# Attention quarters of the next batch grouped 2 + 1 + 2 between the token-mixing groups, on one Trainium2 core

## The chip, the core and the metric

The kernel runs on one core of one Trainium2 chip. The metric is the device time of one execution in microseconds (us), as the median of several runs. The engines are TensorE (matmuls and transposes, its weight loads shown apart), VectorE, ScalarE, GpSimd, and SyncE, which issues the DMAs.

## The reference, cut to what matters

All arrays are float32: batch 8, 8 heads, 576 tokens, 64 channels a head, so 512 channels for a token.

```python
kv = einsum('bhsd,bhse->bhde', k, v)      # per head: k^T v, 64 x 64
out = einsum('bhsd,bhde->bhse', q, kv)
x = out / sqrt(mean(out**2, -1) + 1e-6) * g_norm        # -> (8, 576, 512)

theta = x @ w_theta
y = w_tok_r @ (x * cos(theta)) + w_tok_i @ (x * sin(theta))    # over the tokens
u = x + y
x2 = u + relu(u @ w_ch)

u2 = x2 + (relu(x2^T @ w_tok1) @ w_tok2)^T
return u2 + relu(u2 @ w_ch1) @ w_ch2
```

The change concerns the part down to x2.

## The kernel before, in words

The program has four phases. Phase a computes x2, one batch after the other; phases b, c and d compute the rest, and nothing in them is changed. The five engines run their own instruction lists in order and meet at semaphores. Each list is written out by hand in a function of phase a: `tensor`, `scalar`, `vector`, `gpsimd`, `sync`. What stands where in these lists is the schedule; there is no planner. Matmuls of two kinds occur: the large products run on operands that are split into a high and a low part (three products each, lines 43 to 45 and 367, 368, 373), and the attention and the transposes run on plain fp32 (a quarter's four matmuls have eight records in the profile, a transpose's four have four).

The 576 tokens of a batch are five tiles: four of 128 and one of 64. In what follows **quarter** j (0 to 4) is the attention of one such tile for all heads, `attend(n, j)`: four matmuls (line 312) into a PSUM bank `ps_out[j % 2]`, so quarters 0, 2 and 4 share one bank and 1 and 3 the other. It waits until `norm(n, j - 2)` has read its bank.

For batch b (1 to 6 are the steady ones, written once as a loop body on TensorE) TensorE does:
- `theta(b, 0..4)`: 4 x 12 matmuls and 8 for the last tile, and then `kv(b + 1)`.
- The first half of the token mixing, four groups of output at once, in five pairs of input tiles (`token_mix_first_half`). After the fourth pair comes quarter 0 of batch b + 1.
- Groups five to eight of the token mixing (`token_mix(b, g)`, g = 4 to 7), 27 products each, each followed by one quarter of batch b + 1: quarters 1, 2, 3, 4.
- Eight groups of channel mixing (`channel_mix(b, g)`), 12 products each; `x_transpose(b + 1, 0)` after g = 4 and `x_transpose(b + 1, 1)` after g = 6, the other three behind g = 7. Groups from g = 4 on wait until `relu_add(b, g - 4)` has emptied their bank (that is, `d_x2`).

A quarter is followed by this chain for each tile: `squares` on ScalarE (line 552) into the only `square` tile; `mean_square` on VectorE, a TENSOR_REDUCE (line 721) and a small TENSOR_SCALAR (line 725); the power -1/2 on GpSimd (`inverse_rms`, line 948); `norm` on VectorE (line 733), which reads the quarter's bank; the gain on GpSimd (line 956); later `x_transpose` on TensorE, `x_hi` on ScalarE (line 559) and `x_lo` on VectorE (line 744). `squares(n, j)` waits until the reduction of tile j - 1 has read the `square` tile.

Between these, VectorE does for each token-mixing group g of batch b a `residual(b, g)` (lines 790 and 792; it empties the group's bank and waits for the group to be done) and, once ScalarE has made the high part (`u_hi`, line 596), `u_lo(b, g)` (line 797); and for each channel-mixing group `relu_add(b, g)` (line 805). `turn_q` (line 715) transposes the queries of a later batch, `turn_x2` (line 815) the finished x2.

Of the kernel before, what the change touches and what calls it, by code (L numbers as in the profile page):

```python
# [65 lines left out]
def phase_a(ctx, nc, m, banks, q, k, v, g_norm, w_theta, w_tok_r, w_tok_i, w_ch, x2_dram, x2t_dram):  # L66
    B, H, S, D = q.shape
    DM = H * D
    NC = DM // P
    NJ = 4  # L70
# [3 lines left out]
    NG = 2 * NC  # L74
# [193 lines left out]
    def tensor(pe, nxt):  # L268
# [123 lines left out]
        def token_mix_first_half(b, first):  # L392


            pe.wait_ge(d_frac, NT * b + NJ)
            wait(pe, d_x2, NG * b)
            for pair in range(NT):
                token_mix_pair(b, pair, FIRST_HALF)
                if pair == (1 if first else NJ - 1):
                    attend(b + 1, 0)  # L400

        def token_mix(b, g):

# [81 lines left out]
        def body(b, first=False, more=True):  # L485
            if not first:
                for j in range(NT):
                    theta(b, j)
            if more:
                kv(b + 1)  # L490
                if first:
                    q_transpose(b + 1, 0)
            if first:
                pe.wait_ge(a_whi, 3)
                pe.wait_ge(a_wt, 2 * NT)
                pe.wait_ge(d_wt, 2 * NT + 1)
            if more:
                token_mix_first_half(b, first)
                if first:
                    q_transpose(b + 1, 1)  # L500
                for g in range(NC, NG):
                    token_mix(b, g)
                    attend(b + 1, g - 3)
                    if first and g < NG - 1:
                        q_transpose(b + 1, g - 2)
            else:
                token_mix_last()
            if first:
                pe.wait_ge(d_wlo, 3)
            for g in range(NG):  # L510
                channel_mix(b, g)
                if more and g == 4:
                    x_transpose(b + 1, 0)
                if more and g == 6:
                    x_transpose(b + 1, 1)
            if more:
                for j in range(2, NT):
                    x_transpose(b + 1, j)
# [14 lines left out]
    def scalar(act, nxt):  # L533
# [15 lines left out]
        def squares(n, j):  # L549
            act.wait_ge(p_out, NT * n + j + 1)  # L550
            wait(act, d_ss, NT * n + j)
            act.activation(square, ps_out[j % 2][:, :], ACT.Square).then_inc(a_sq, 1)  # L552
# [82 lines left out]
        def body(b, first=False, more=True):  # L635
            if first:

                for j in range(NT):
                    if j + 1 < NT:
                        x_hi(0, j + 1)  # L640
                    if j == NJ:
                        turn_left(0)
                    tok_weight_hi(NT + 1 + j)
                    if 1 <= j <= 3:
                        sines(0, j - 1)
                tok_weight_hi(2 * NT + 1)
                act.wait_ge(a_left, 4)
                act.activation(wtok[0][:, 2 * NJ, :], left_tok[:, :], ACT.Copy).then_inc(a_whi, 1)
                act.wait_ge(d_wlo, 2)
                z_hi(0, 0)  # L650
                sines(0, 3)
                z_hi(0, 1)
                q_copy(1, 0)
                z_hi(0, 2)
                z_hi(0, 3)
                act.wait_ge(s_raw[2], DMA)
                act.activation(wch[0][:, :, :], raw_ch[:, :, :], ACT.Copy).then_inc(a_whi, 1)
                sines(0, NJ)
                z_hi(0, NJ)
            else:  # L660
                sines(b, 0)
                z_hi(b, 0)
                sines(b, 1)
                sines(b, 2)
                z_hi(b, 1)
                sines(b, 3)
                turn_left(b)
                if more:
                    kv_copy(b + 1)
                z_hi(b, 2)  # L670
                z_hi(b, 3)
                sines(b, NJ)
                z_hi(b, NJ)
            if more:
                squares(b + 1, 0)
            for g in range(NG):
                u_hi(b, g)
                if first and g == 0:
                    q_copy(b + 1, 1)
                if more and g >= NC:  # L680
                    squares(b + 1, g - 3)
                    if first and g < NG - 1:
                        q_copy(b + 1, g - 2)
            if more:
                for j in range(NT):
                    x_hi(b + 1, j)
            else:
                nxt["weights_hi"](act)
                act.wait_ge(g_zlo, NK * B)
                act.wait_ge(d_z, 2 * NT * B)  # L690
                for piece in range(3):
                    nxt["x_hi"](act, 0, piece)
        body(0, first=True)
        for b in range(1, B - 1):
            body(b)
# [3 lines left out]
    def vector(dve, nxt):  # L699
# [155 lines left out]
        def body(b, first=False, more=True):  # L855
            if first:

                for j in range(NT):
                    if 2 <= j + 1 < NT:
                        x_lo(0, j + 1)  # L860
                    if j >= 2:
                        rotate(0, j - 2)
                    if j < 3:
                        fraction(0, j)
                        magnitude(0, j)
                    if j == NJ:
                        fraction(0, 3)
                        magnitude(0, 3)
                    tok_weight_lo(NT + 1 + j)
                tok_weight_lo(2 * NT + 1)  # L870
                dve.wait_ge(a_whi, 3)
                dve.tensor_tensor(wtok[1][:, 2 * NJ, :], left_tok[:, :], wtok[0][:, 2 * NJ, :].bitcast(F32),
                                  ALU.subtract).then_inc(d_wt, 1)
                kv_copy(1)
                rotate(0, 3)
                fraction(0, NJ)
                magnitude(0, NJ)
                rotate(0, NJ)
                dve.wait_ge(a_whi, 4)
                dve.tensor_tensor(wch[1][:, :, :], raw_ch[:, :, :], wch[0][:, :, :].bitcast(F32),  # L880
                                  ALU.subtract).then_inc(d_wlo, 1)
            else:
                for j in range(NJ):
                    fraction(b, j)
                    magnitude(b, j)
                    if j >= 1:
                        rotate(b, j - 1)
                rotate(b, NJ - 1)
                fraction(b, NJ)
                magnitude(b, NJ)  # L890
                if more:
                    for hp in range(EARLY_TURNS, HP):
                        turn_q(b + 1, hp)
                rotate(b, NJ)
            if first:
                dve.wait_ge(d_wlo, 3)
            if more:
                mean_square(b + 1, 0)
            for g in range(NG):
                if more and g > NC:  # L900
                    norm(b + 1, g - NC)
                residual(b, g)
                if g >= 1:
                    u_lo(b, g - 1)
                if more and g >= NC:
                    mean_square(b + 1, g - 3)
                if more and g == 2:
                    norm(b + 1, 0)
            u_lo(b, NG - 1)
            for g in range(NG):  # L910
                relu_add(b, g)
                if more and g > NC:
                    turn_x2(b, g - NC - 1, turned)
                if more and g == 0:
                    norm(b + 1, NT - 1)
                if 1 <= g <= EARLY_TURNS and 1 <= b < B - 2:
                    turn_q(b + 2, g - 1)
                if first and g in (NC, NC + 2):
                    turn_q(b + 2, g // 2 - 2)
                if more and g == 5:  # L920
                    x_lo(b + 1, 0)
                if not more and g == 3:
                    nxt["weights_lo"](dve)
                if not more and g == 5:
                    nxt["x_lo"](dve, 0, 0)
                if not more and g == 6:
                    turn_x2(b, 0, turned_last)
            if more:
                for j in range(1, NT):
                    x_lo(b + 1, j)  # L930
                turn_x2(b, NC - 1, turned)
            else:
                nxt["x_lo"](dve, 0, 1)
                nxt["x_lo"](dve, 0, 2)
                for c in range(1, NC):
                    turn_x2(b, c, turned_last)
# [1297 lines left out]
```

## Time and profile before

| what | us |
|---|---|
| median of 3 runs | 1176.63 (1175.86 to 1177.12) |
| the profiled execution's own time | 1176.91 |
| its span in the profile | 1175.1 |
| TensorE busy | 1154.3 (98% of the span) |
| VectorE busy | 834.9 (71%) |
| ScalarE busy | 481.0 (41%) |
| GpSimd busy | 327.9 (28%) |

The span runs from the first to the last instruction of the program in one profiled execution; its own time is 1.8 us longer, for what lies around it. Phase a takes the first 485 us or so of it. Engines are named PE (TensorE's matmuls), PEld (its weight loads), DVE (VectorE), ACT (ScalarE), POOL (GpSimd) and SP (SyncE). A row of the timeline gives the start, the duration from the start of the first to the end of the last of the instructions merged in it, the engine and line, the operation, what it writes and reads, its shape, and their number. The ends of matmuls are modelled, so that neighbouring rows overlap.

### The profile page before, as it was taken

Reading aid. Unit: us, or ns where it says so; the run is one execution under the profiler, and the core shown is the slowest. Engines: PE = TensorE matmul, PEld = TensorE weight load, DVE = VectorE, ACT = ScalarE, POOL = GpSimd, SP = SyncE. Lnnn points to the kernel's source line nnn. Section 1 sums busy time; section 2 is a strip of 40 time slices with the busy share of each in tenths; the row PEclk is TensorE's granted clock in tenths of the full one; section 3 lists DMA queues with packets and bytes.
Section 4 is the critical chain, followed back from the end, with each engine's and each line's share of the span. In section 5 each row is a group of like instructions: output and inputs, shape, how many; then the busy total and the mean of one; then the engine's idle time right before and its main releaser. Section 6 shows DMA issues by size and latency. Waiting matters only on the chain.

```text
span 1175.1 us, 20563 instructions
## 1 busy us (share of the span) xinstructions
PE 1154.3 (98%) x7790; PEld 1116.7 (95%) x7790; DVE 834.9 (71%) x1243; ACT 481.0 (41%) x758; POOL 327.9 (28%) x210
## 2 busy tenths in 40 slices
PE   5999999999999999999999999999999999999998
PEld 5799999999999999999988999999999999999998
DVE  3968878686969687777557667667666786666664
ACT  3623425141424233334343555555556543333331
POOL 4462434444353534331552313214200000000000
PEclk9999999999999999999999999999999999999999
DMA  9714526160625330319997888666768999999983
GB/s 278 197 28 107 122 69 133 44 144 13 164 38 149 52 80 0 83 42 303 332 310 279 280 310 272 266 238 242 286 229 312 397 300 293 262 252 307 296 207 54
DMA packets 327383, 228.25 MB, mean 194 GB/s; under 512 B 231440, under 2 KB 295312, under 8 KB 326288
## 3 DMA queue, kind: packets, MB, share of 16 engines
q1 hardware_dynamic: 324912, 227.03, 63.3%
q8 instruction: 42, 0.69, 0.2%
q10 hardware_dynamic: 2400, 0.30, 0.2%
q14 instruction: 29, 0.24, 0.1%
HBM read 136.84 MB, written 92.80 MB: 195 GB/s over the span
## 4 chain that ended last, share of the span: by engine, by line
PE 86%; DMA 5%; DVE 3%; SPq 2%; issue 1%; POOL 1%; ACT 1%; DVEq 0%; ACTq 0%; POOLq 0%
PE bank L43 10%; PE bank L45 10%; PE bank L44 10%; PE bank L1377 10%; PE bank L1379 10%; PE bank L1378 10%; PE bank L367 6%; PE bank L373 6%; PE bank L368 6%; DMA u_scratch<-attention_u 3%; PE bank L312 3%; PE bank L326 1%; PE bank L282 1%; DMA attention_g<-g_scratch 1%; DVE attention_u L1268 1%
## 5 line engine op out<-in xcount | busy, mean ns | idle before, releaser
L367 PE MATMUL bank<-weights_tok,z_z 128*128 128x288 f32 x576 | 164.3, 300 | 0.3
L368 PE MATMUL bank<-weights_tok,z_z 128*128 128x288 f32 x576 | 161.2, 294 | 0.0
L373 PE MATMUL bank<-weights_tok,z_z 128*128 128x288 f32 x576 | 125.0, 295 | 0.8 <-POOL z_z L965 0.6
L367 PEld LDWEIGHTS bank<-weights_tok,z_z 128*128 128x128 f32 x576 | 108.1, 188 | 1.2 <-issue 1.1
L368 PEld LDWEIGHTS bank<-weights_tok,z_z 128*128 128x128 f32 x576 | 108.1, 188 | 0.0
L948 POOL TENSOR_TENSOR weights_rms_inverse<-weights_mean_squares,weights_minus_half 128x8 f32<-128x8 f32 x40 | 66.4, 1662 | 114.2 <-DVE weights_mean_squares L725 114.0
L373 PEld LDWEIGHTS bank<-weights_tok,z_z 128*128 128x128 f32 x576 | 92.5, 187 | 1.3 <-POOL z_z L965 0.8
L596 ACT ACTIVATE weights_x_channel_major<-attention_u 128x288 fp32r<-128x288 f32 x64 | 28.5, 446 | 139.0 <-DVE attention_u L792 139.0
L43 PE MATMUL bank<-weights_x_channel_major,weights_ch 128*128 128x288 f32 x256 | 77.4, 302 | 0.0
L963 POOL TENSOR_TENSOR z_z<-tokens_cos,z_z 128x512 fp32r<-128x512 f32 x24 | 31.9, 1329 | 159.8 <-ACT z_z L589 143.8
L45 PE MATMUL bank<-weights_x_channel_major,weights_ch 128*128 128x288 f32 x256 | 75.4, 294 | 0.0
L44 PE MATMUL bank<-weights_x_channel_major,weights_ch 128*128 128x288 f32 x256 | 75.4, 294 | 0.0
L1610 ACT ACTIVATE attention_staged<-bank 128x384 f32<-128x384 f32 x108 | 52.5, 490 | 33.7 <-PE bank L1379 31.9
L1377 PE MATMUL bank<-z_u_slot,weights_up 128*128 128x384 f32 x192 | 64.1, 334 | 0.0
L1378 PE MATMUL bank<-z_u_slot,weights_up 128*128 128x384 f32 x192 | 64.1, 334 | 0.0
L1379 PE MATMUL bank<-z_u_slot,weights_up 128*128 128x384 f32 x192 | 64.1, 334 | 0.0
L721 DVE TENSOR_REDUCE weights_sum_squares<-weights_fraction 128x8 f32<-128x512 f32 x40 | 27.4, 686 | 35.2 <-ACT weights_fraction L552 35.0
L1664 DVE TENSOR_TENSOR attention_staged<-attention_staged 128x384 f32<-128x384 f32 x36 | 31.5, 874 | 27.4 <-ACT attention_staged L1610 27.3
L43 PEld LDWEIGHTS bank<-weights_x_channel_major,weights_ch 128*128 128x128 f32 x256 | 48.0, 188 | 1.6 <-issue 1.2
L43 PE MATMUL bank<-weights_theta,weights_x_channel_major 128*128 128x512 f32 x124 | 49.2, 397 | 0.0
L45 PE MATMUL bank<-weights_theta,weights_x_channel_major 128*128 128x512 f32 x124 | 48.4, 390 | 0.0
L44 PE MATMUL bank<-weights_theta,weights_x_channel_major 128*128 128x512 f32 x124 | 48.3, 389 | 0.0
(297 smaller groups left out, 3589.7 us busy)
## 6 DMA issues: line engine op xcount, KB each, us to landing
g_scratch<-attention_staged SPq DMA_DIRECT2D x36, 960.0 KB, 3.9
weights_g<-g_scratch SPq DMA_DIRECT2D x24, 1152.0 KB, 10.6
g_scratch<-attention_staged SPq DMA_DIRECT2D x36, 384.0 KB, 4.7
x_scratch<-attention_u SPq DMA_DIRECT2D x8, 1152.0 KB, 4.5
u_scratch<-attention_u SPq DMA_DIRECT2D x16, 576.0 KB, 7.6
weights_raw_u<-u_scratch SPq DMA_DIRECT2D x6, 1536.0 KB, 7.7
qkv_u_left<-u_scratch SPq DMA_DIRECT2D x12, 768.0 KB, 10.1
x_tokens_scratch<-z_x_turned SPq DMA_DIRECT2D x112, 72.0 KB, 2.0
```

Source lines behind the costliest of these rows:

```text
L43: eng.matmul(out, w[0], x[0], start=first, stop=False)
L44: eng.matmul(out, w[0], x[1], start=False, stop=False)
L45: return eng.matmul(out, w[1], x[0], start=False, stop=last)
L312: mm = pe.matmul(ps_out[j % 2][0:rows(j), hp * P:(hp + 1) * P], qt[:, hp, j * P:j * P + rows(j)], kvbd[hp // 2][:, hp % 2, :], start=True, ...
L367: pe.matmul(out, x, wtok[0][:, zt, hs], start=(i == 0), stop=False)
L368: pe.matmul(out, x, wtok[1][:, zt, hs], start=False, stop=False)
L373: mm = pe.matmul(tok_bank(b, g)[:, 0:HALF], z[1][:, zt, c * P:(c + 1) * P], wtok[0][:, zt, half * HALF:(half + 1) * HALF], start=False, st ...
L948: gp.tensor_tensor(rms_inv[:, i, :], msq[:, i, :], minus_half[:, :], ALU.pow).then_inc(g_pow, 1)
L1377: eng.matmul(out, w[0], x[0], start=False, stop=False, skip_group_check=True)
L1378: eng.matmul(out, w[0], x[1], start=False, stop=False, skip_group_check=True)
L1379: return eng.matmul(out, w[1], x[0], start=False, stop=last, skip_group_check=True)
L1610: act.activation(tile(n, k), src, ACT.Relu).then_inc(done, 1)
```

## The change

In the steady batches (b = 1 to 6) the quarters of the next batch get other places. Quarter 1 stands right behind quarter 0, after the fourth pair; quarter 2 behind group five (g = 4); quarters 3 and 4 behind group eight (g = 7). ScalarE's squares and VectorE's mean squares and norms are moved along: `mean_square(1)` now stands ahead of the first `residual`, `norm(1)` behind `residual(3)`, `mean_square(2)` behind `residual(5)`, `norm(2)` ahead of `residual(6)`, `mean_square(3)` and `(4)` behind the last `u_lo`, and `norm(3)` and `(4)` behind the first two `relu_add`. Batch 0 keeps its order of quarters. In batches 0 to 6, `x_transpose(b + 1, 0)` moves from behind channel group g = 4 to g = 6, where the transpose of tile 1 stands, and `x_lo(b + 1, 0)` from g = 5 to g = 6.

```diff
@@ -398,6 +398,8 @@
                 token_mix_pair(b, pair, FIRST_HALF)
                 if pair == (1 if first else NJ - 1):
                     attend(b + 1, 0)
+                if pair == NJ - 1 and not first:
+                    attend(b + 1, 1)
 
         def token_mix(b, g):
 
@@ -500,18 +502,23 @@
                     q_transpose(b + 1, 1)
                 for g in range(NC, NG):
                     token_mix(b, g)
-                    attend(b + 1, g - 3)
-                    if first and g < NG - 1:
-                        q_transpose(b + 1, g - 2)
+                    if first:
+                        attend(b + 1, g - 3)
+                        if g < NG - 1:
+                            q_transpose(b + 1, g - 2)
+                    elif g == NC:
+                        attend(b + 1, 2)
+                    elif g == NG - 1:
+                        attend(b + 1, 3)
+                        attend(b + 1, 4)
             else:
                 token_mix_last()
             if first:
                 pe.wait_ge(d_wlo, 3)
             for g in range(NG):
                 channel_mix(b, g)
-                if more and g == 4:
+                if more and g == 6:
                     x_transpose(b + 1, 0)
-                if more and g == 6:
                     x_transpose(b + 1, 1)
             if more:
                 for j in range(2, NT):
@@ -673,14 +680,21 @@
                 z_hi(b, NJ)
             if more:
                 squares(b + 1, 0)
+                if not first:
+                    squares(b + 1, 1)
             for g in range(NG):
                 u_hi(b, g)
+                if more and not first and g == NC:
+                    squares(b + 1, 2)
                 if first and g == 0:
                     q_copy(b + 1, 1)
-                if more and g >= NC:
+                if first and g >= NC:
                     squares(b + 1, g - 3)
-                    if first and g < NG - 1:
+                    if g < NG - 1:
                         q_copy(b + 1, g - 2)
+            if more and not first:
+                squares(b + 1, 3)
+                squares(b + 1, 4)
             if more:
                 for j in range(NT):
                     x_hi(b + 1, j)
@@ -896,28 +910,41 @@
                 dve.wait_ge(d_wlo, 3)
             if more:
                 mean_square(b + 1, 0)
+                if not first:
+                    mean_square(b + 1, 1)
             for g in range(NG):
-                if more and g > NC:
+                if first and g > NC:
                     norm(b + 1, g - NC)
+                if more and not first and g == NC + 2:
+                    norm(b + 1, 2)
                 residual(b, g)
                 if g >= 1:
                     u_lo(b, g - 1)
-                if more and g >= NC:
+                if first and g >= NC:
                     mean_square(b + 1, g - 3)
+                if more and not first and g == 3:
+                    norm(b + 1, 1)
+                if more and not first and g == NC + 1:
+                    mean_square(b + 1, 2)
                 if more and g == 2:
                     norm(b + 1, 0)
             u_lo(b, NG - 1)
+            if more and not first:
+                mean_square(b + 1, 3)
+                mean_square(b + 1, 4)
             for g in range(NG):
                 relu_add(b, g)
                 if more and g > NC:
                     turn_x2(b, g - NC - 1, turned)
-                if more and g == 0:
+                if first and g == 0:
                     norm(b + 1, NT - 1)
+                if more and not first and g < 2:
+                    norm(b + 1, 3 + g)
                 if 1 <= g <= EARLY_TURNS and 1 <= b < B - 2:
                     turn_q(b + 2, g - 1)
                 if first and g in (NC, NC + 2):
                     turn_q(b + 2, g // 2 - 2)
-                if more and g == 5:
+                if more and g == 6:
                     x_lo(b + 1, 0)
                 if not more and g == 3:
                     nxt["weights_lo"](dve)
```

TensorE, a steady batch, from the last low products of the fourth pair to the next quarters (line 312 is a quarter, lines 367, 368 and 373 are token mixing). Before:

```order
L373 MATMUL bank<-weights_tok,z_z 128x288 x8
L312 MATMUL bank<-attention_kv_blockdiag_0,attention_q_transposed 128x128 x2
L312 MATMUL bank<-weights_kv_blockdiag_0,attention_q_transposed 128x128 x2
L367 MATMUL bank<-weights_tok,z_z 128x288
L368 MATMUL bank<-weights_tok,z_z 128x288
...
L373 MATMUL bank<-weights_tok,z_z 128x288
L312 MATMUL bank<-attention_kv_blockdiag_0,attention_q_transposed 128x128 x2
L312 MATMUL bank<-weights_kv_blockdiag_0,attention_q_transposed 128x128 x2
L367 MATMUL bank<-weights_tok,z_z 128x288
```

After:

```order
L373 MATMUL bank<-weights_tok,z_z 128x288 x8
L312 MATMUL bank<-attention_kv_blockdiag_0,attention_q_transposed 128x128 x2
L312 MATMUL bank<-weights_kv_blockdiag_0,attention_q_transposed 128x128 x2
L312 MATMUL bank<-attention_kv_blockdiag_0,attention_q_transposed 128x128 x2
L312 MATMUL bank<-weights_kv_blockdiag_0,attention_q_transposed 128x128 x2
L367 MATMUL bank<-weights_tok,z_z 128x288
L368 MATMUL bank<-weights_tok,z_z 128x288
...
L373 MATMUL bank<-weights_tok,z_z 128x288
L312 MATMUL bank<-attention_kv_blockdiag_0,attention_q_transposed 128x128 x2
L312 MATMUL bank<-weights_kv_blockdiag_0,attention_q_transposed 128x128 x2
L367 MATMUL bank<-weights_tok,z_z 128x288
```

The first quarter is now followed by a second one at once. Behind the rest of the first half and group five there stood quarter 1 before, and there stands quarter 2 now.

VectorE, the same place in the program (before: line 721 and 725 are the mean square, 790 and 792 a residual, 797 a low part, 733 a norm). Before:

```order
L721 TENSOR_REDUCE weights_sum_squares<-weights_fraction 128x8
L725 TENSOR_SCALAR weights_mean_squares<-weights_sum_squares 128x8
L790 TENSOR_TENSOR attention_u<-bank,weights_x_channel_major 128x288
L792 TENSOR_TENSOR attention_u<-attention_u,weights_x_channel_major 128x288
...
L797 TENSOR_TENSOR weights_x_channel_major<-attention_u,weights_x_channel_major 128x288
L733 TENSOR_TENSOR attention_x_normed_0<-bank,weights_rms_inverse 128x512
L790 TENSOR_TENSOR attention_u<-bank,weights_x_channel_major 128x288
```

After, with the line numbers of the changed kernel (735, 739, 804, 806, 811 and 747 in the same order of meaning):

```order
L735 TENSOR_REDUCE weights_sum_squares<-weights_fraction 128x8
L739 TENSOR_SCALAR weights_mean_squares<-weights_sum_squares 128x8
L735 TENSOR_REDUCE weights_sum_squares<-weights_fraction 128x8
L739 TENSOR_SCALAR weights_mean_squares<-weights_sum_squares 128x8
L804 TENSOR_TENSOR attention_u<-bank,weights_x_channel_major 128x288
L806 TENSOR_TENSOR attention_u<-attention_u,weights_x_channel_major 128x288
...
L811 TENSOR_TENSOR weights_x_channel_major<-attention_u,weights_x_channel_major 128x288
L747 TENSOR_TENSOR attention_x_normed_0<-bank,weights_rms_inverse 128x512
L804 TENSOR_TENSOR attention_u<-bank,weights_x_channel_major 128x288
```

A second mean square stands ahead of the first residual. The norm of tile 0 keeps its place between the low part of the second group and the residual of the fourth.

## Rows read from the trace of the kernel before

**Rows 1.** The page: busy us (share of span) xinstructions; the chain that ended last, by engine.

```profile
PE 1154.3 (98%) x7790; PEld 1116.7 (95%) x7790; DVE 834.9 (71%) x1243; ACT 481.0 (41%) x758; POOL 327.9 (28%) x210
...
PE 86%; DMA 5%; DVE 3%; SPq 2%; issue 1%; POOL 1%; ACT 1%; DVEq 0%; ACTq 0%; POOLq 0%
```

**Rows 2.** Timeline of TensorE: quarter 0 in two batches (start us, us, engine, line, operation).

```profile
195.24 0.60 PE L312 MATMUL bank<-attention_kv_blockdiag,attention_q_transposed 128*128 128x128 f32 x4
...
259.15 0.61 PE L312 MATMUL bank<-attention_kv_blockdiag,attention_q_transposed 128*128 128x128 f32 x4
```

**Rows 3.** Timeline of TensorE: the rest of the first half, quarter 1 and what follows.

```profile
197.31 0.55 PE L373 MATMUL bank<-weights_tok,z_z 128*128 128x288 f32 x3
...
201.30 0.61 PE L312 MATMUL bank<-attention_kv_blockdiag,attention_q_transposed 128*128 128x128 f32 x4
...
202.11 0.38 PE L367 MATMUL bank<-weights_tok,z_z 128*128 128x288 f32 x1
202.32 0.30 PE L368 MATMUL bank<-weights_tok,z_z 128*128 128x288 f32 x1
```

**Rows 4.** Timeline of TensorE: batch 0, a quarter with four transposes behind it.

```profile
72.25 0.61 PE L312 MATMUL bank<-attention_kv_blockdiag,attention_q_transposed 128*128 128x128 f32 x4
...
73.14 0.60 PE L297 MATMUL bank<-const_ident,qkv_q 128*128 128x128 f32 x4
73.49 0.38 PE L367 MATMUL bank<-weights_tok,z_z 128*128 128x288 f32 x1
73.71 0.30 PE L368 MATMUL bank<-weights_tok,z_z 128*128 128x288 f32 x1
```

**Rows 5.** Timeline of TensorE: three transposes in one run, and the next product.

```profile
229.69 1.47 PE L326 MATMUL bank<-const_ident,tokens_x_token_major 128*128 128x128 f32 x12
230.91 0.48 PE L43 MATMUL bank<-weights_theta,weights_x_channel_major 128*128 128x512 f32 x1
```

**Rows 6.** Timeline of TensorE: quarter 4, of 64 rows, and the next product.

```profile
214.87 0.65 PE L312 MATMUL bank<-attention_kv_blockdiag,attention_q_transposed 128*64 128x128 f32 x4
...
215.88 0.40 PE L43 MATMUL bank<-weights_x_channel_major,weights_ch 128*128 128x288 f32 x1
```

**Rows 7.** Timeline of ScalarE: the squares of quarter 0.

```profile
196.33 0.60 ACT L552 ACTIVATE weights_fraction<-bank 128x512 f32<-128x512 f32 x1 [0.81 <-PE bank L312]
```

**Rows 8.** Timeline of VectorE: mean square, first residual, norm of quarter 0.

```profile
196.96 0.69 DVE L721 TENSOR_REDUCE weights_sum_squares<-weights_fraction 128x8 f32<-128x512 f32 x1 [2.11 <-ACT weights_fraction L552]
197.68 0.17 DVE L725 TENSOR_SCALAR weights_mean_squares<-weights_sum_squares 128x8 f32<-128x8 f32 x1
197.79 0.46 DVE L790 TENSOR_TENSOR attention_u<-bank,weights_x_channel_major 128x288 f32<-128x288 f32 x1
...
201.12 0.68 DVE L733 TENSOR_TENSOR attention_x_normed<-bank,weights_rms_inverse 128x512 f32<-128x512 f32 x1
```

**Rows 9.** Timeline of all engines: a quarter at the program's start that waits for ScalarE.

```profile
19.75 0.60 ACT L537 ACTIVATE attention_q_transposed<-bank 128x512 f32<-128x512 f32 x1
...
20.40 0.52 PEld L312 LDWEIGHTS bank<-attention_kv_blockdiag,attention_q_transposed 128*128 128x128 f32 x4 [0.93 <-ACT attention_q_transposed L537]
20.43 0.68 PE L312 MATMUL bank<-attention_kv_blockdiag,attention_q_transposed 128*128 128x128 f32 x4 [0.72 <-ACT attention_q_transposed L537]
...
21.40 0.27 PE L459 MATMUL bank<-const_ident,z_raw_tok 128*128 128x128 f32 x1
```

**Rows 10.** Timeline of all engines: transpose 0, and the relu_add that group 5 needs.

```profile
223.84 0.45 DVE L805 SCALAR_TENSOR_TENSOR attention_u<-bank,attention_u 128x288 f32<-128x288 f32 x1
223.91 0.60 PE L326 MATMUL bank<-const_ident,tokens_x_token_major 128*128 128x128 f32 x4
...
224.34 0.40 PE L43 MATMUL bank<-weights_x_channel_major,weights_ch 128*128 128x288 f32 x1
```

**Rows 11.** Timeline of GpSimd: the power of quarter 1.

```profile
205.86 1.64 POOL L948 TENSOR_TENSOR weights_rms_inverse<-weights_mean_squares,weights_minus_half 128x8 f32<-128x8 f32 x1 [6.29 <-DVE weights_mean_squares L725]
```

**Rows 12.** Windows, 12 to 36 us: length; busy PE, PEld, DVE, ACT, POOL; clock; DMA.

```profile
12.00:36.00 24.00, 18.02 (x130) 14.91 (x127) 16.61 (x31) 12.39 (x23) 15.15 (x10) 1.00 1.12 322
```

## The prediction

> **What bounds the kernel now.** I read the page's busy shares first, then the chain of waits, then the timeline of one steady batch on each engine, and at last the granted clock. TensorE is busy for 98% of the span and its own work is 86% of the chain that ended last, while VectorE has 71% [rows 1]. So an instruction on another engine costs nothing until TensorE stands before a semaphore because of it, and whatever TensorE waits is added to the span in full. Busy time cannot show a short wait, because the ends of matmuls are modelled and overlap; I therefore read starts. The six steady batches (b = 1 to 6) are alike: attention quarter 0 starts at 195.24 us in the second of them and at 259.15 us in the third, 63.91 us later [rows 2]. I work in the batch of 195.24 us and multiply by six. Batches 0 and 7 keep their order, but for the place of one transpose in batch 0.
>
> **Term 1: five short runs become three (0).** The change takes attention quarters 1 and 3 out of runs of their own and joins them to quarters 0 and 4. A quarter alone takes 0.81 us (201.30 to 202.11) and the mixing product behind it takes a step of 0.21 us, where such a step is otherwise 0.13 (three products in 0.55 us, less the last's own 0.29, are two steps): 0.89 in all [rows 3]. Is a joined quarter cheaper? Batch 0 has joined runs: there the quarter takes 0.89 us (72.25 to 73.14), the four transposes behind it 0.35, and the step after them is 0.22 [rows 4]. A joined quarter costs 0.89 too: what a lone run loses in its first step after, it had gained at its end. The same holds for the transposes: a run that ends with four takes 0.35 us for them, twelve together 1.22 us [rows 4, 5], and the difference of 0.87 for eight is 0.109 each, so a run of four is 0.44 by its members and 0.35 + 0.09 (the excess of the step behind it) by its rows: nothing is left over for the run itself. Joining transposes 0 and 1 therefore also brings 0. The last quarter, of 64 rows, is dearer: 1.01 us instead of 0.81 [rows 3, 6]. It stays so; it only follows a quarter now and not a product. No row shows that pair, so I take 0 and keep 0.1 us a batch on both sides, half of what sets this quarter apart.
>
> **Term 2: quarter 2 comes to a wait (+6.7 us).** Quarter 2 overwrites the bank of quarter 0, so it waits for `norm(0)` on VectorE. Before, that wait was long over: `norm(0)` ran at 201.12 [rows 8], and quarter 2 came a whole group behind quarter 1. Now one quarter is put ahead, and nothing between it and quarter 2 but the rest of the first half and group five. TensorE arrives where quarter 1 stood, one quarter later: 201.30 + 0.89 = 202.19 us [rows 3].
> When does `norm(0)` end? VectorE is in order, and `mean_square(1)` now stands ahead of the first `residual`. Step by step, from the rows: `squares(0)` on ScalarE runs 196.33 to 196.93 [rows 7], the reduction starts 0.03 later, at 196.96, and ends at 197.65 [rows 8]. There is one `square` tile, so `squares(1)` can start only then: 197.68 to 198.28. Its reduction starts at 198.31 and its small TENSOR_SCALAR 0.72 later, as in the row pair 196.96 and 197.68, at 199.03. Before, the TENSOR_SCALAR ahead of the first residual started at 197.68 [rows 8]. All of VectorE's work behind it moves by 1.35 us. Its three residuals and two low parts up to `norm(0)` ran without idle time in 3.33 us (197.79 to 201.12) and are the same instructions now. So `norm(0)` starts at 202.47 and, at 0.68 us, ends at 203.15.
> TensorE wakes a little after. The nearest row is the start of the program: the copy on ScalarE ends at 19.75 + 0.60 = 20.35, and the waiting quarter's matmul starts at 20.43, 0.08 later; that run of eight then takes 0.97 us to 21.40, against 0.89 [rows 4, 9], another 0.08. The wait is 203.15 + 0.08 - 202.19 = 1.04, with the restart 1.12 us a batch, 6.7 us for six.
> Here a rule of the Trainium skill would say otherwise. In those rows the weight load itself starts at 20.40, after the release and not before it [rows 9]. The page "TensorE: Matmul & The Clock Gate", section "Part 2: What happens when you issue a matmul", says that TensorE pulls weight loads ahead of matmuls in flight; if it did so ahead of this wait as well, the restart's 0.08 us would be saved, 1.04 instead of 1.12 us a batch, and the sum would be +5.7. The measured rows decide here, so I keep 1.12.
>
> **Term 3: a small wait goes (-0.5 us).** Transpose 0 stood behind channel group g = 4, and group g = 5 behind it needs `relu_add(1)`. That one is late: it stands behind `norm(4)`, starts at 223.84 and ends at 224.29, and the product starts at 224.34 [rows 10]. The transpose run thus takes 0.43 us (223.91 to 224.34) against the 0.35 of four others [rows 4]: 0.08 us a batch. In the new order `relu_add(1)` stands ahead of `norm(4)` and waits for nothing but its product. -0.08 x 6 = -0.5 us.
>
> **Term 4: what is now late elsewhere, and covered (0).** Each is followed with the shift of 1.1 us. `norm(2)` gates quarter 4: group six ends near 208.0, a residual with a low part is 1.2 us (three and two of them are the 3.33 above), a mean square 0.83 (196.96 to 197.79) [rows 8], GpSimd's power 1.64 [rows 11]; `norm(2)` is done by 212.5, and quarter 4 comes at 215.9 (203.3, two quarters of 0.9 and three groups of 27 steps of 0.133, 3.6 each). Cover 3.4 us. The first `residual` moves 1.35 us, and group six needs its bank only at 204.2. Quarters 3 and 4 end at 217.0; their squares and sums fill VectorE to 219.3, the two powers, with a gain between them that I take as long [rows 11], end at 222.9, `norm(4)` at 223.6, a query turn and `relu_add(2)` a little over 1 us later, at 224.8. Channel group g = 6 needs that one at 217.0 + 6 x 1.6 = 226.6 (a group is twelve products of 0.133). Cover 1.8 us. On ScalarE and GpSimd nothing is added, and no DMA is moved past another: SP's stores and loads wait for semaphores whose last increments keep their places.
>
> **Sum:** +6.7 - 0.5 = +6.2 us. The profiled execution took 1176.9 us (span 1175.1) and lies 0.3 above the median of the runs, 1176.63; the sum on the median gives **1182.8 us**. A measurement of this kernel can tell about 0.2%, 2.4 us, from no change.
>
> **Rivals.**
> *A short wait.* If the extra sum on VectorE cost nothing, the first residual would still have to wait for group one, whose last product (one step ahead of the 197.31 row) ends near 197.47, now 0.89 later, 198.36. With 3.33, 0.68 and 0.08 that is 202.45: a wait of 0.26, with the restart 0.34 us, and 6 x 0.34 - 0.5 = +1.5 us: 1178.1 [rows 3, 8]. For it: VectorE had 2.11 us idle just ahead of this place. Against it: that idle time lies before `squares(0)` ended [rows 8], so it cannot take work that depends on it. Chance 0.09.
> *Faster.* If leaving and entering an fp32 run does cost something that the lone runs' early end hides, every run joined saves up to the step's excess of 0.09; three runs a batch fewer are 6 x 0.27 = 1.6 us, with term 3 2.1 us: 1174.5. It decides only where the wait of term 2 is under 0.35 us a batch, and rows 4 and 5 speak against it. Chance 0.06.
> *The clock falls.* The granted clock is 1.00, the 2.4 GHz level, also between 12 and 36 us [rows 12], where TensorE waited 0.7 us at once [rows 9] and was busy for 18 of 24 us. If the new idle time brought it to 1.2 GHz for about one group in each batch, the 3.6 us of that group would double: +22 us, 1204. The Trainium skill's page "TensorE: Matmul & The Clock Gate", section "A second HAM failure mode: psum-queue depth-cycling", describes frequent short idle times of TensorE that make the clock go back and forth; by it this rival could hold, and no row here shows it. Chance 0.02.
> *The change adds no wait:* the order allows it only if VectorE's part before `norm(0)` were 1 us shorter than its rows. I count that with the short wait.
>
> **How the numbers follow.** The forecast has 0.83. Its own range is 0.96 to 1.34 us a batch in term 2 (wake and restart between none and twice the rows, and at the top 0.03 us more at each of the two hand-overs between ScalarE and VectorE), and the last quarter's 0.1 on both sides: 5.8 - 0.5 - 0.6 = +4.7 to 8.0 - 0.5 + 0.6 = +8.1, so 1181.3 to 1184.7. To leave out no more than 2 in 10 I take the low end down to the short wait: **1178.1 to 1184.7**. Slower by over 0.2%: 0.85 (forecast and clock). Within 0.2%: 0.08. Faster: 0.07.
>
> **What would show it.** In the chain or the waits of TensorE there must be a new entry: the matmul of quarter 2 waiting for VectorE's norm, six times, about 1.0 us each. The distance between two batches' quarter 0 must be 64.95 us instead of 63.91. VectorE must show the second reduction near +3.1 us after the start of quarter 0 and `norm(0)` at +7.2. Term 1 is right if a pair of quarters takes 1.7 us to the next product; term 3 if a pair of transposes takes 0.79. The prediction is wrong if that wait is absent, if its length is under 0.4 us, or if a second wait stands at quarter 4 or in the channel groups.

## The result, and the profile after

| | before | with the change |
|---|---|---|
| median of 6 runs, us | 1176.71 (1175.86 to 1177.25) | 1183.20 (1182.32 to 1183.71) |
| span of the profiled execution, us | 1175.1 | 1181.5 |
| from one batch's quarter 0 to the next one's, us | 63.91 | 65.02 |

The ratio is 1.0055 with a 95% interval of 1.0045 to 1.0066: slower by 6.5 us, where +6.2 us was forecast. The distance of two batches grew by 1.11 us, and six of them make 6.7 us, which is the whole difference within the scatter of the runs. So it lies in the steady batches of phase a.

The page of the profile gives busy time and share of the span, and hardly shows the difference (compare [rows 1]): TensorE is still at 98%.

```profile
PE 1157.0 (98%) x7790; PEld 1119.1 (95%) x7790; DVE 835.4 (71%) x1243; ACT 481.8 (41%) x758; POOL 328.9 (28%) x210
```

The waits of TensorE, restricted to the steady part (100 to 485 us), name the cause (the engine and line that waited, for whom: us in total, times, longest):

```profile
PE bank L312 <- DVE attention_x_normed L747: 5.4, 6, 0.9
```

In the kernel before this list was empty in the same stretch. The clock is the same as before; a window of the changed kernel (length; busy PE, PEld, DVE, ACT, POOL; granted clock; share and GB/s of the DMA):

```profile
100.00:490.00 390.00, 384.27 (x3050) 365.29 (x3049) 311.85 (x522) 132.57 (x258) 162.08 (x114) 1.00 0.35 82
```

In the list of waits, line 747 is `norm` (733 before). The list gives 0.9 us for each wait, which is less than what it costs, since it counts from the modelled end of the last matmul. The starts tell the price. TensorE in the batch that answers to [rows 2, 3] (quarters 0 and 1, the product behind them, quarter 2, the product behind it), and quarter 0 of the next batch:

```profile
196.41 0.61 PE L312 MATMUL bank<-attention_kv_blockdiag,attention_q_transposed 128*128 128x128 f32 x4
...
198.12 0.38 PE L367 MATMUL bank<-weights_tok,z_z 128*128 128x288 f32 x1
...
204.44 0.71 PE L312 MATMUL bank<-attention_kv_blockdiag,attention_q_transposed 128*128 128x128 f32 x4 [0.90 <-DVE attention_x_normed L747]
...
205.36 0.38 PE L367 MATMUL bank<-weights_tok,z_z 128*128 128x288 f32 x1
...
261.43 0.60 PE L312 MATMUL bank<-attention_kv_blockdiag,attention_q_transposed 128*128 128x128 f32 x4
```

The first product behind quarters 0 and 1 starts at 198.12. In the kernel before, the first product behind quarter 0 was this row:

```profile
196.04 0.38 PE L367 MATMUL bank<-weights_tok,z_z 128*128 128x288 f32 x1
```

From there to the next quarter, at 201.30 [rows 3], it was 5.26 us, so quarter 2 could now have come at 203.38. It came at 204.44: 1.06 us late. Its run, from its start to the next product's start at 205.36, took 0.92 us instead of the 0.81 of a quarter that did not wait: another 0.11, called the slow restart below. The wait costs 1.17 us a batch. The rows of ScalarE and of VectorE that lead to it, answering to [rows 7, 8]:

```profile
197.50 0.60 ACT L559 ACTIVATE weights_fraction<-bank 128x512 f32<-128x512 f32 x1 [0.83 <-PE bank L312]
198.92 0.60 ACT L559 ACTIVATE weights_fraction<-bank 128x512 f32<-128x512 f32 x1 [0.82 <-DVE weights_sum_squares L735]
```

```profile
198.13 0.69 DVE L735 TENSOR_REDUCE weights_sum_squares<-weights_fraction 128x8 f32<-128x512 f32 x1 [2.12 <-ACT weights_fraction L559]
198.86 0.17 DVE L739 TENSOR_SCALAR weights_mean_squares<-weights_sum_squares 128x8 f32<-128x8 f32 x1
199.55 0.69 DVE L735 TENSOR_REDUCE weights_sum_squares<-weights_fraction 128x8 f32<-128x512 f32 x1 [0.52 <-ACT weights_fraction L559]
200.27 0.17 DVE L739 TENSOR_SCALAR weights_mean_squares<-weights_sum_squares 128x8 f32<-128x8 f32 x1
200.38 0.46 DVE L804 TENSOR_TENSOR attention_u<-bank,weights_x_channel_major 128x288 f32<-128x288 f32 x1
...
203.71 0.68 DVE L747 TENSOR_TENSOR attention_x_normed<-bank,weights_rms_inverse 128x512 f32<-128x512 f32 x1
```

The second reduction starts at 199.55, 3.14 us behind the start of quarter 0, `norm(0)` starts at 203.71, 7.30 us behind it, and ends at 204.39; TensorE starts 0.05 later. `squares(1)` starts only when the first reduction has ended (198.82), and VectorE stands idle for 0.52 us until the squares are there.

The other three places. TensorE at quarters 3 and 4 and at the joined transposes, answering to [rows 6, 10]:

```profile
216.11 0.29 PE L373 MATMUL bank<-weights_tok,z_z 128*128 128x288 f32 x1
216.24 0.61 PE L312 MATMUL bank<-attention_kv_blockdiag,attention_q_transposed 128*128 128x128 f32 x4
...
217.22 0.65 PE L312 MATMUL bank<-attention_kv_blockdiag,attention_q_transposed 128*64 128x128 f32 x4
...
218.24 0.40 PE L43 MATMUL bank<-weights_x_channel_major,weights_ch 128*128 128x288 f32 x1
...
229.47 1.03 PE L326 MATMUL bank<-const_ident,tokens_x_token_major 128*128 128x128 f32 x8
230.26 0.38 PE L43 MATMUL bank<-weights_x_channel_major,weights_ch 128*128 128x288 f32 x1
```

Quarter 3 takes 0.98 us before the narrow quarter 4, 0.09 more than a joined one of 0.89, and the 64-row quarter 1.02, as before. Before, it was the product ahead of quarter 4 whose step was 0.09 too long: it started at 214.65 and quarter 4 at 214.87 [rows 6], a step of 0.22 where 0.13 is usual.

```profile
214.65 0.29 PE L373 MATMUL bank<-weights_tok,z_z 128*128 128x288 f32 x1
```

The first weight load of that quarter, in the same kernel, starts with its matmul:

```profile
214.87 0.41 PEld L312 LDWEIGHTS bank<-attention_kv_blockdiag,attention_q_transposed 128*64 128x64 f32 x4 [0.16 <-issue]
```

So the price of the narrow quarter went over to its new neighbour and is the same. The two transposes take 0.79 us, and no wait is left in the channel groups.

### The profile page after: what moved, and what is told of

The parts are those of the page before. It is cut to its first block, busy times and chain, and to the rows that moved or that the text cites. A ratio compares the mean times of both kernels' runs of the same rounds, so it can differ in the third digit from the quotient of the medians.

```text
span 1181.5 us, 20563 instructions
## 1 busy us (share of the span) xinstructions
PE 1157.0 (98%) x7790; PEld 1119.1 (95%) x7790; DVE 835.4 (71%) x1243; ACT 481.8 (41%) x758; POOL 328.9 (28%) x210
## 4 chain that ended last, share of the span: by engine, by line
PE 88%; DVE 5%; DMA 3%; POOL 1%; ACT 1%; issue 1%; SPq 0%; ACTq 0%; POOLq 0%
PE bank L43 11%; PE bank L45 11%; PE bank L44 11%; PE bank L1406 11%; PE bank L1404 11%; PE bank L1405 11%; PE bank L367 5%; PE bank L373 5%; PE bank L368 5%; PE bank L312 3%; DMA u_scratch<-attention_u 3%; PE bank L282 1%; PE bank L326 1%; DVE attention_u L1295 1%; DVE weights_sum_squares L735 1%
## 5 line engine op out<-in xcount | busy, mean ns | idle before, releaser
L566 ACT ACTIVATE weights_x_channel_major<-bank 128x512 fp32r<-128x512 f32 (+1 forms) x40 | 20.8, 557 | 81.1 <-PE bank L326 81.1
```

## The experiments

The tables and texts use the distance from one batch's quarter 0 to the next one's, because it repeats within 0.03 us in an execution, while whole runs differ by more than 1 us. Each ratio is against runs of the kernel before that were taken beside it.

| kernel | us a batch, expected | us a batch, measured | median us (before beside it) | ratio, 95% interval |
|---|---|---|---|---|
| before | | 63.91 | 1176.71 | |
| the change | 64.95 | 65.02 | 1183.20 | 1.0055 (1.0045 to 1.0066) |
| norm0_early | 63.85 | 63.85 | 1176.12 (1176.32) | 1.0002 (0.9993 to 1.0011) |
| sum1_late | 64.2 | 64.22 | 1178.14 (1176.32) | 1.0021 (1.0012 to 1.0031) |
| two_squares | 64.5 | 64.50 | 1179.82 (1176.32) | 1.0031 (1.0019 to 1.0043) |
| transposes_only | 64.3 | 64.35 | 1178.94 (1176.32) | 1.0022 (1.0011 to 1.0032) |
| norm4_late | 63.82 | 63.82 | 1175.09 (1176.41) | 0.9988 (0.9979 to 0.9997) |
| transposes_back | 65.02 | 65.02 | 1182.70 (1176.41) | 1.0050 (1.0035 to 1.0066) |

**norm0_early: take the wait away, keep everything else.** From the changed kernel:

```diff
@@ vector, the loop over the token-mixing groups
-                if more and g == 2:
+                if first and g == 2:
                     norm(b + 1, 0)
+                if more and not first and g == 0:
+                    norm(b + 1, 0)
```

> The changed kernel with norm(0) moved up on VectorE, from behind residual(2) to behind residual(0). Theory (the whole loss is quarter 2 waiting for norm(0)): norm(0) ends about 1.5 us before quarter 2 comes, the wait of 1.17 us a batch (1.07 plus 0.10 restart in the trace of the change) goes, the distance between two batches' quarter 0 falls from 65.02 to about 63.85 us, and the time is that of before less some 0.4 us: 1176.3, ratio 0.9997. Rival (joining the runs or the pair of quarters 3 and 4 costs something itself): over 64.0 us a batch and over 1177.5 us though no wait is left at quarter 2. Rival (leaving fewer fp32 runs saves time): under 63.7 us a batch, under 1175.5.

Measured: 63.85 us a batch and no wait of TensorE between 100 and 485 us. Its timeline of TensorE (quarter 2) and of VectorE (`norm(0)`):

```profile
195.22 0.61 PE L312 MATMUL bank<-attention_kv_blockdiag,attention_q_transposed 128*128 128x128 f32 x4
...
202.19 0.61 PE L312 MATMUL bank<-attention_kv_blockdiag,attention_q_transposed 128*128 128x128 f32 x4
```

```profile
200.05 0.69 DVE L747 TENSOR_TENSOR attention_x_normed<-bank,weights_rms_inverse 128x512 f32<-128x512 f32 x1
```

`norm(0)` ends at 200.74, and quarter 2 starts at 202.19, 6.97 us behind quarter 0, with its run at the ordinary pace. The weight loads of quarter 2, in the changed kernel, where it waits, and in norm0_early, where it does not:

```profile
204.44 0.52 PEld L312 LDWEIGHTS bank<-attention_kv_blockdiag,attention_q_transposed 128*128 128x128 f32 x4 [1.13 <-DVE attention_x_normed L747]
```

```profile
202.06 0.54 PEld L312 LDWEIGHTS bank<-attention_kv_blockdiag,attention_q_transposed 128*128 128x128 f32 x4
```

Behind the wait the first load starts with its matmul; without the wait it starts 0.13 us ahead of it. Moving one VectorE instruction ahead of two residuals and two low parts gives back 1.17 us a batch. What is left of the change costs or saves next to nothing: 63.85 against 63.91 is 0.06 us less, while the small wait of term 3 alone is worth 0.09 (norm4_late, below, takes 63.82 without it), so 0.03 us a batch is left for all the joined runs. The rival that joined runs save up to 0.27 us a batch is out, and so is the one that they cost enough to explain the loss.

**sum1_late: the other half of the cause.** From the changed kernel:

```diff
@@ vector
             if more:
                 mean_square(b + 1, 0)
-                if not first:
-                    mean_square(b + 1, 1)
...
                 if more and g == 2:
                     norm(b + 1, 0)
+                    if not first:
+                        mean_square(b + 1, 1)
```

> The changed kernel with mean_square(1) moved from ahead of the first residual to behind norm(0). Theory (two parts of the wait: the extra sum on VectorE, and that quarter 2 comes one quarter's time earlier against the residuals, which must wait for the groups): the first residual starts when group one is done, norm(0) ends near quarter 0 plus 7.1 us, and quarter 2 waits 0.26 us, 0.34 with the restart; 64.2 us a batch and 1178.1 us. Rival (the sum alone makes the wait): no wait, 63.85 us a batch, 1176.3. Rival (the sum has no part in it): the wait stays over 1 us, 1183.

Measured: 64.22 us a batch. VectorE:

```profile
197.43 0.17 DVE L739 TENSOR_SCALAR weights_mean_squares<-weights_sum_squares 128x8 f32<-128x8 f32 x1
198.17 0.46 DVE L804 TENSOR_TENSOR attention_u<-bank,weights_x_channel_major 128x288 f32<-128x288 f32 x1 [0.56 <-PE bank L373]
...
201.49 0.68 DVE L747 TENSOR_TENSOR attention_x_normed<-bank,weights_rms_inverse 128x512 f32<-128x512 f32 x1
```

and TensorE, quarter 0 and quarter 2:

```profile
194.99 0.61 PE L312 MATMUL bank<-attention_kv_blockdiag,attention_q_transposed 128*128 128x128 f32 x4
...
202.23 0.71 PE L312 MATMUL bank<-attention_kv_blockdiag,attention_q_transposed 128*128 128x128 f32 x4
```

Without the second sum, VectorE waits 0.56 us for group one (the row of the first residual says so), and `norm(0)` ends at 202.17, 7.18 us behind quarter 0 at 194.99. Quarter 2 starts at 202.23, 7.24 us behind it instead of 6.97: 0.27 us late, 0.37 with its slow restart (64.22 against the 63.85 of norm0_early). That is the prediction's short wait, 0.34. So two things make the wait of 1.17: 0.80 us comes with the sum put ahead of the residuals (it delays them by less than the 1.41 us that it takes up, since they would have waited 0.56 for group one), and 0.37 is there without it, because quarter 2 now comes a whole group sooner while group one, which the first residual waits for, ends one quarter's time later.

**two_squares: a smaller dose of the same.** The squares of odd quarters get a tile of their own (`square` is `frac[:, 0, :]`, and they go into `frac[:, 1, :]`), so that ScalarE does not wait for the reduction of the quarter before:

```diff
@@ scalar, squares(n, j)
-            wait(act, d_ss, NT * n + j)
-            act.activation(square, ps_out[j % 2][:, :], ACT.Square).then_inc(a_sq, 1)
+            wait(act, d_ss, NT * n + (max(j - 1, 0) if n > 1 else j))
+            act.activation(frac[:, j % 2, :], ps_out[j % 2][:, :], ACT.Square).then_inc(a_sq, 1)
@@ vector, mean_square(n, j)
-            dve.tensor_reduce(ssum[:, i, :], square.rearrange("p (h e) -> p h e", h=H),
+            dve.tensor_reduce(ssum[:, i, :], frac[:, i, :].rearrange("p (h e) -> p h e", h=H),
...
```

> The changed kernel with two tiles for the squares, by the parity of the quarter, so that squares(1) does not wait until the first reduction has read its tile. Theory (the wait follows VectorE's chain one to one): VectorE loses its 0.52 us of idle time between the two sums, norm(0) ends 0.52 us earlier and the wait at quarter 2 falls by as much; 64.5 us a batch, 3.1 us below the changed kernel, 1180.1. Rival (quarter 2 waits for something else than VectorE's order, such as GpSimd's power): the wait stays, 1183.

Measured: 64.50 us a batch, 0.52 less than the change. VectorE and TensorE:

```profile
197.39 0.69 DVE L735 TENSOR_REDUCE weights_sum_squares<-weights_fraction 128x8 f32<-128x512 f32 x1 [2.11 <-ACT weights_fraction L559]
198.11 0.17 DVE L739 TENSOR_SCALAR weights_mean_squares<-weights_sum_squares 128x8 f32<-128x8 f32 x1
198.29 0.69 DVE L735 TENSOR_REDUCE weights_sum_squares<-weights_fraction 128x8 f32<-128x512 f32 x1
...
202.44 0.68 DVE L747 TENSOR_TENSOR attention_x_normed<-bank,weights_rms_inverse 128x512 f32<-128x512 f32 x1
```

```profile
195.67 0.61 PE L312 MATMUL bank<-attention_kv_blockdiag,attention_q_transposed 128*128 128x128 f32 x4
...
203.18 0.71 PE L312 MATMUL bank<-attention_kv_blockdiag,attention_q_transposed 128*128 128x128 f32 x4 [0.39 <-DVE attention_x_normed L747]
```

The second reduction follows the first sum without idle time, `norm(0)` starts 6.77 us behind quarter 0 instead of 7.30, and quarter 2 starts 7.51 us behind it instead of 8.03. VectorE's chain and TensorE's wait move together, 0.53 and 0.52 us. The row of `norm(0)` has no idle time ahead of it: it waits for its place in VectorE's list, not for GpSimd's power.

**transposes_only: the second part of the change by itself.** From the kernel before:

```diff
@@ tensor
-                if more and g == 4:
-                    x_transpose(b + 1, 0)
                 if more and g == 6:
+                    x_transpose(b + 1, 0)
                     x_transpose(b + 1, 1)
@@ vector
-                if more and g == 5:
+                if more and g == 6:
                     x_lo(b + 1, 0)
```

> The kernel before with one part of the change: transpose 0 and its low part moved from behind channel group g = 4 to g = 6. Theory (relu_add(1), late behind norm(4), ends at 224.29 whatever TensorE does, and the transposes filled that time): group g = 5 still starts at 224.34, now out of a wait of 0.4 us, and the transposes are done again later for 0.44: about 0.35 to 0.43 us a batch more, 64.3 us a batch, 1178.7 to 1179.3. Rival (the move itself saves the 0.08 us of term 3): 63.85 us a batch, 1176.2.

Measured: 64.35 us a batch, +0.44, and a ratio of 1.0022. TensorE at the step into channel group g = 5, and VectorE ahead of it:

```profile
224.33 0.29 PE L45 MATMUL bank<-weights_x_channel_major,weights_ch 128*128 128x288 f32 x1
224.89 0.40 PE L43 MATMUL bank<-weights_x_channel_major,weights_ch 128*128 128x288 f32 x1 [0.26 <-DVE attention_u L804]
```

```profile
223.78 0.69 DVE L732 TENSOR_TENSOR attention_x_normed<-bank,weights_rms_inverse 128x512 f32<-128x512 f32 x1 [1.16 <-POOL weights_rms_inverse L947]
224.39 0.45 DVE L804 SCALAR_TENSOR_TENSOR attention_u<-bank,attention_u 128x288 f32<-128x288 f32 x1
```

`relu_add(1)` (here line 804) ends at 224.84 behind `norm(4)`, and the product starts at 224.89, 0.56 us behind the last one instead of 0.13: 0.43 us. The transposes had stood in that gap; moved away, they leave it empty and are done later, where they add 0.44. In the kernel before the small wait looked like 0.08 us because 0.35 us of transposes covered the rest. In the whole change this loss does not show, since its VectorE part takes `norm(4)` out of the way.

**norm4_late: the small wait alone, from the kernel before.**

```diff
@@ vector, the loop over the channel-mixing groups
-                if more and g == 0:
+                if more and g == (0 if first else 1):
                     norm(b + 1, NT - 1)
```

> The kernel before with one move on VectorE in the steady batches: norm(4) from behind relu_add(0) to behind relu_add(1). Theory (the small wait of channel group g = 5 is relu_add(1) standing behind norm(4)): the step into group g = 5 comes 0.08 to 0.10 us earlier, 63.82 us a batch, 0.5 us below before: 1176.2. Rival (the transpose run is slower at that place for another reason): 63.91 us a batch, no difference.

Measured: 63.82 us a batch, 0.09 less, and 1175.09 against 1176.41 us. The step into group g = 5, and VectorE:

```profile
223.50 0.60 PE L326 MATMUL bank<-const_ident,tokens_x_token_major 128*128 128x128 f32 x4
223.85 0.38 PE L43 MATMUL bank<-weights_x_channel_major,weights_ch 128*128 128x288 f32 x1
```

```profile
221.19 0.82 DVE L805 SCALAR_TENSOR_TENSOR attention_u<-bank,attention_u 128x288 f32<-128x288 f32 x2
222.81 0.69 DVE L733 TENSOR_TENSOR attention_x_normed<-bank,weights_rms_inverse 128x512 f32<-128x512 f32 x1 [0.79 <-POOL weights_rms_inverse L948]
```

The transpose run takes 0.35 us now instead of 0.43 [rows 10]; both `relu_add` are done before `norm(4)`. This kernel is the one version here whose interval lies below that of before: 0.9979 to 0.9997. By the batch distance the gain is 0.09 x 6 = 0.5 us; the 1.3 us between the medians is more than that, and the rest is not explained by the trace; the interval allows 0.5 as well.

**transposes_back: is there anything in joining the two transposes?** From the changed kernel, transpose 0 and its low part go back behind g = 4 and g = 5:

```diff
@@ tensor
+                if more and g == 4:
+                    x_transpose(b + 1, 0)
                 if more and g == 6:
-                    x_transpose(b + 1, 0)
                     x_transpose(b + 1, 1)
@@ vector
-                if more and g == 6:
+                if more and g == 5:
                     x_lo(b + 1, 0)
```

> The changed kernel with transpose 0 and its low part back behind channel group g = 4. Theory (runs of transposes have no cost of their own, and relu_add(1) is early in the new order): 65.02 us a batch as with the change, 1183.2, and the step into group g = 5 without a wait. Rival (joining the two transposes saved the 0.08 us): 65.1 us a batch, 1183.7.

Measured: 65.02 us a batch, the same as with the change, and 1182.70 us. The transpose run at its old place:

```profile
225.83 0.60 PE L326 MATMUL bank<-const_ident,tokens_x_token_major 128*128 128x128 f32 x4
226.18 0.38 PE L43 MATMUL bank<-weights_x_channel_major,weights_ch 128*128 128x288 f32 x1
```

It takes 0.35 us there. Two runs or one, the transposes cost the same.

## Why the prediction was right

- **Which wait ends last.** The forecast was that nothing but a new wait of quarter 2 for `norm(0)` would count. It is the only wait of TensorE in the steady part, six times, and norm0_early removes it and with it the whole loss. Term by term the distance of two batches comes out: 1.17 for the wait, -0.09 for term 3 and 0.03 for all the rest make the 1.11 us that it grew by. Each term came out near its forecast, so that the total is not right by large errors that cancelled.
- **Term 1 (0).** Right. A joined quarter takes 0.89 us (two of them 1.71, from 196.41 to 198.12), joined transposes 0.79, and the 64-row quarter keeps its price. norm0_early leaves 0.03 us a batch for all of it; the transposes' part of it is 0.00 by transposes_back.
- **Term 2 (1.12 us a batch).** It measured 1.17. The arrival of quarter 2 was forecast at 6.95 us behind quarter 0 and would have been 6.97. `norm(0)` was forecast at +7.23 and came at +7.30: the step that was mis-sized is the hand-over of VectorE to ScalarE, from the end of the first reduction to `squares(1)`, 0.10 us where the prediction took 0.03 from the hand-over the other way (and allowed 0.03 more in its range). TensorE started 0.05 us behind the release instead of 0.08, and the slow restart was 0.11 instead of 0.08: these two small errors cancel, by luck, and 0.05 us a batch is left: 0.07 from the hand-over less the 0.02 by which TensorE came later.
- **The rule on weight loads that was weighed against the rows.** The Trainium skill's page "TensorE: Matmul & The Clock Gate", section "Part 2: What happens when you issue a matmul", says that weight loads are pulled ahead of matmuls in flight; by that rule carried over the wait, the restart would have been saved. The trace does not show it there: the waiting quarter's first load starts with its matmul at 204.44, behind the release, where norm0_early has it 0.13 us ahead, and the run takes 0.92 us instead of 0.81.
- **Term 3 (-0.08 us a batch).** Its cause was right (norm4_late: -0.09), its account was incomplete. The prediction took the wait to be 0.08 us long; transposes_only shows that it costs 0.43 us as soon as no transposes stand in it. The term came out because the change moves `norm(4)` as well, as the prediction said.
- **Term 4 (covered).** Right: no second wait appeared. `norm(4)` starts 27.5 us behind quarter 0 (223.88), where 27.7 was forecast (222.9 on the anchor of 195.24); `relu_add(2)` ends at 225.60, and channel group g = 6 begins near 227.87 (twelve steps of 0.133 ahead of the transposes at 229.47). The cover is 2.3 us, 1.8 was forecast.
- **The rivals.** The short wait exists, as sum1_late shows, but as a part of the long one. Nothing was gained by fewer fp32 runs. The clock did not fall: from 100 to 490 us the granted clock is 1.00, the 2.4 GHz level, through a wait of 1.1 us in each of the six batches. The Trainium skill's page "TensorE: Matmul & The Clock Gate", section "A second HAM failure mode: psum-queue depth-cycling", describes frequent short idle times that make the clock go back and forth; for waits like these the trace does not agree.

## What to carry to other kernels

On an engine that is never idle, regrouping independent work brings nothing if each piece costs the same in both places; what remains is the set of waits, and for each of them two sums from one anchor (when the waiter comes, when the releaser ends) gave 1.12 us a batch where 1.17 was measured. When a piece is moved ahead, look at what moves ahead with it in the in-order list of the helping engine: here the sum that belongs to quarter 1 came to stand in front of the norm that quarter 2 needs. And work that stands in front of a late wait covers it, so that moving it away can cost as much as it takes (+0.44 us a batch in transposes_only).

## What the runs showed of the hardware that was not expected

- A hand-over from VectorE to ScalarE took 0.10 us (reduction ends at 198.82, squares start at 198.92), that from ScalarE to VectorE 0.03 us (the first squares end at 198.10, the reduction starts at 198.13).
- TensorE starts 0.05 us after the end of VectorE's `norm(0)` (204.39 to 204.44), but its first run after the wait is slower by 0.11 us: the first four records take 0.71 us (204.44) where an unhindered run's take 0.61. The first weight load then starts with its matmul and not 0.13 us ahead of it.
- The change from 128 to 64 columns of weights costs 0.09 us ahead of it, whether a 288-column product stands there (a step of 0.22 instead of 0.13, before) or an fp32 quarter (0.98 instead of 0.89, with the change). The narrow quarter keeps this price with its new neighbour. Its first weight load starts together with its matmul, as the one behind the wait does. That this is the reason for the 0.09 us is not shown.
